# Moving a PSUM copy ahead of an absolute value on ScalarE, and VectorE's half of an outer product directly behind a difference

## The chip, the cores and the metric

The program runs on one core of a Trainium2 chip. The metric is the device time of one execution in microseconds; three executions of the kernel before were timed and one more was profiled.

## The reference

Three stages follow each other on 6016 tokens (two batches of 3008) of width 256:

```python
X = np.fft.fft(np.fft.fft(x, axis=1), axis=2).real      # x: (2, 3008, 256)
h = X.reshape(6016, 256) @ w_in1;  g = np.maximum(h, 0.0) ** 2;  z = g @ w_out1    # w_in1: (256, 2048)
h = z @ w_in2                                                                       # w_in2: (256, 2048)
P = a[0] + a[1] * h + a[2] * h**2 + a[3] * h**3
Q = 1.0 + np.abs(b[0]) * np.abs(h) + np.abs(b[1]) * h**2
out = (P / (Q + 1e-6)) @ w_out2                                                     # (6016, 256)
```

## The kernel before

**Stages.** The first 70 us or so transform the input: a DFT in two factors (`stage1`, `stage3`), with the DFT over the width folded into the first weight matrix. From there on the kernel is one pipeline of STEPS = 96 steps. The tokens are columns; a tile holds 256 column pairs (k and its mirror image), which are 512 columns of the output, and there are 12 tiles, the last one narrower (196 pairs, 392 columns). Each tile has 8 units of the hidden width, a unit being two blocks of 128 of the 2048 hidden features. A step handles one unit in each of four matrix products, skewed against each other: in step s, TensorE does `up1(s)` (first layer up), `down1(s - 2)`, `up2(s - 10)` (second layer up) and `down2(s - 12)`. Every product is done with values split in a high and a low part (`_hi`, `_lo`), three matmuls for one.

**The first layer and its mirror image.** For the column k and its mirror image the hidden value is a plus part plus or minus a minus part. `up1` computes the minus part into one PSUM bank (`h1_minus`, L901) and the plus part into another (`h1_plus`, L909). The plus part has one more term, an outer product of a row of the transform (`u_s`) with a weight column (`w_col`), which is not computed by TensorE: it is written into the plus bank first, and TensorE's plus matmuls add to it. The bank holds two blocks of 256 columns. In the first 12 steps (SHARED = SKEW + 2 = 12) VectorE writes both blocks (L707); afterwards ScalarE writes the second (L555) and VectorE the first. PSUM has one plus bank and one minus bank, so the outer product of unit s + 1 can be written only when VectorE has read the plus bank of unit s (`diff_done`).

**ScalarE's order in a step s** (from step 12 on; every operation is 128 partitions x 1024 columns unless another size is given): relu (L562) and square (L564) of unit s; its half of the outer product of s + 1 (L555, 256 columns); at the end of a tile, the high part of z (L619); |v| (L580) and the cubic term (L588) of the second layer's unit s - 10, both read from PSUM; the high part of g1 (`keep_hi1`, L571); at the end of a tile, the copy of the output out of PSUM (L626); |q'| (`abs_q`, L594), which needs VectorE's q'; the copy of the minus part of unit s + 1 (`keep_minus`, L547, 512 columns); the natural logarithm (L604) and the exponential (L607), which make the seed of the reciprocal of Q. The logarithm waits for |q'| by a semaphore, the exponential for the logarithm.

**VectorE's order in a step s**: sum (L735) and difference (L736) of unit s, from the plus bank and the copied minus part, 512 columns each; the division of unit s - 11 (`divide`: L753, L755, L759, the first one waits for the seed); its half of the outer product of s + 1 (L707); at the end of a tile, the low part of z (L764); then `read_h2` of unit s - 10 (L742 makes the signed q' and waits for ScalarE's two results; L743 and L745 make the polynomial and free the PSUM banks of `up2`).

**GpSimd's order**: high (L501) and low part (L503) of the divided g2, then the low part of g1 (`keep_lo1`, L494).

Every engine runs its program in the order written, and stands still at a wait. The waits that the change touches: VectorE's outer product waited for ScalarE's half of the same unit (`act_outer_ready`), ScalarE's for the difference of the unit before; TensorE's plus matmuls waited for VectorE's half (`outer_ready`), and so for both. The DMAs of these steps (the tile's inputs from DRAM, the output) are issued by SyncE's queue once per tile.

Of the kernel before, what the change touches and what calls it, by code (L numbers as in the profile page):

```python
# [64 lines left out]
SHARED = SKEW + 2  # L65
# [67 lines left out]
def fft_moe_kernel(nc, x, w_in1, w_out1, w_in2, w_out2, coef, f47, fold, twiddle, pair, out_t):  # L133
# [9 lines left out]
    with ctx:  # L143
# [105 lines left out]
        def unit(m):  # L249

            return m if 0 <= m < STEPS else None
# [265 lines left out]
        def _(act):  # L517
# [31 lines left out]
            def outer_product(m):  # L549
                t, n = m // UNITS, pairs(m // UNITS)  # L550
                f = 2 * (m % UNITS) + 1
                if m % UNITS == 0:
                    act.wait_ge(u_loaded[t % Y_BUFS], 16 * (t // Y_BUFS + 1))
                act.wait_ge(diff_done, m)
                nc.scalar.activation(h1_plus(m)[:, 1, :], u_s[:, t % Y_BUFS, 0:n], ACT.Copy, scale=w_col[:, f:f + 1]  # L555
                                     ).then_inc(act_outer_ready, 1)

# [82 lines left out]
            for s in range(STEPS):  # L640
                second, summed, multiplied = unit(s - SKEW), unit(s - LAG1), unit(s - SKEW - LAG2)
                square_relu(s)
                if SHARED <= s + 1 < STEPS:
                    outer_product(s + 1)
                if summed is not None and summed % UNITS == UNITS - 1:
                    keep_z_hi(summed // UNITS)
                if second is not None:
                    from_h2(second)
                if s >= HEAD:
                    keep_hi1(s)  # L650
                if multiplied is not None and multiplied % UNITS == UNITS - 1:
                    keep_out(multiplied // UNITS)
                if second is not None:
                    abs_q(second)
                if unit(s + 1) is not None:
                    keep_minus(s + 1)
                if s == 0:
                    keep_y_hi(EARLY)
                if second is not None:
                    seed_from_q(second)  # L660
                if s < HEAD:
                    keep_hi1(s)
                if s == 0:
                    keep_y_hi(EARLY + 1)
# [19 lines left out]
        def _(dve):  # L684
# [13 lines left out]
            def outer_product(m):  # L698
                t, n = m // UNITS, pairs(m // UNITS)
                if m % UNITS == 0:  # L700
                    dve.wait_ge(u_loaded[t % Y_BUFS], 16 * (t // Y_BUFS + 1))
                after(dve, diff_done, m)
                if m >= SHARED:
                    dve.wait_ge(act_outer_ready, m + 1 - SHARED)
                for i in range(2 if m < SHARED else 1):
                    f = 2 * (m % UNITS) + i
                    nc.vector.tensor_scalar(h1_plus(m)[:, i, :], u_s[:, t % Y_BUFS, 0:n], w_col[:, f:f + 1], None, ALU.mult  # L707
                                            ).then_inc(outer_ready, 1)
# [68 lines left out]
            for s in range(STEPS):  # L777
                second, before, summed = unit(s - SKEW), unit(s - SKEW - 1), unit(s - LAG1)
                add_and_subtract(s)
                if before is None:  # L780
                    outer_product(s + 1)
                if s == 1:
                    keep_y_lo(EARLY)
# [3 lines left out]
                    keep_y_lo(EARLY + 1)  # L787
                if before is not None:
                    divide(before)
                if before is not None and unit(s + 1) is not None:  # L790
                    outer_product(s + 1)
                if summed is not None and summed % UNITS == UNITS - 1:
                    keep_z_lo(summed // UNITS)
                if second is not None:
# [8 lines left out]
            m = STEPS - 1  # L803
# [10 lines left out]
        def _(pe):  # L814
# [74 lines left out]
            def up1(m):  # L889
# [12 lines left out]
                                                start=(i == 0 and (a, c) == (1, 0)), stop=(a, c) == (0, 0),  # L902
                                                skip_group_check=True)
                last.then_inc(minus_ready, 1)
                pe.wait_ge(outer_ready, 2 * m + 2 if m < SHARED else SHARED + m + 1)
                for i in range(2):
                    f = slice((2 * (m % UNITS) + i) * P, (2 * (m % UNITS) + i + 1) * P)
                    for a, c in ((1, 0), (0, 1), (0, 0)):
# [106 lines left out]
```

## Time and profile before

| | before |
|---|---|
| median of three runs | 1044.67 us (1043.86 to 1045.47) |
| the profiled execution's own time | 1044.86 us |
| its span in the trace | 1043.1 us |
| TensorE matmul / VectorE / ScalarE / GpSimd busy | 1005.7 / 919.0 / 913.4 / 573.0 us |
| granted TensorE clock, mean | 0.995 |

The span runs from the first to the last recorded instruction; the time of the execution is somewhat longer. Busy shares are means over the whole span, and a matmul's end is modelled, so TensorE's busy time does not say how far it is from its own limit. A row of the timeline gives the start of an instruction, its duration, and in brackets how long its engine stood idle before it and for whom. An instruction's recorded duration overlaps with the start of the next one on its engine, so the distance between two starts is what an instruction takes of its engine's time.

### The profile page before, as it was taken

Reading aid. Unit: us, or ns where it says so; the run is one execution under the profiler, and the core shown is the slowest. Engines: PE = TensorE matmul, PEld = TensorE weight load, DVE = VectorE, ACT = ScalarE, POOL = GpSimd, SP = SyncE. Lnnn points to the kernel's source line nnn. Section 1 sums busy time; section 2 is a strip of 40 time slices with the busy share of each in tenths; the row PEclk is TensorE's granted clock in tenths of the full one; section 3 lists DMA queues with packets and bytes.
Section 4 is the critical chain, followed back from the end, with each engine's and each line's share of the span. In section 5 each row is a group of like instructions: output and inputs, shape, how many; then the busy total and the mean of one; then the engine's idle time right before and its main releaser. Section 6 shows DMA issues by size and latency. Waiting matters only on the chain.

```text
span 1043.1 us, 13795 instructions
## 1 busy us (share of the span) xinstructions
PE 1005.7 (96%) x5098; PEld 840.4 (81%) x5098; DVE 919.0 (88%) x956; ACT 913.4 (88%) x1013; POOL 573.0 (55%) x305
## 2 busy tenths in 40 slices
PE   9999899999999999999999999999999999999975
PEld 8798778888888888888888888788788788888864
DVE  2369899999999999999999999989999999999997
ACT  2348899999999999999999999999999999999873
POOL 0246765655655656556556565565565655655352
PEclk9999999999999999999999999999999999999998
DMA  9767000001001001001001001001001000000000
GB/s 259 276 194 232 11 1 26 1 1 47 1 1 46 1 1 46 1 1 46 1 1 46 1 1 46 1 1 46 1 1 40 1 1 21 1 21 1 1 20 16
DMA packets 24992, 38.03 MB, mean 36 GB/s; under 512 B 1743, under 2 KB 19035, under 8 KB 24539
## 3 DMA queue, kind: packets, MB, share of 16 engines
q1 hardware_dynamic: 24876, 37.14, 11.3%
q8 instruction: 40, 0.66, 0.3%
q14 instruction: 28, 0.22, 0.1%
q10 hardware_dynamic: 48, 0.02, 0.0%
HBM read 25.31 MB, written 11.84 MB: 36 GB/s over the span
## 4 chain that ended last, share of the span: by engine, by line
ACT 55%; PE 16%; DVE 16%; issue 11%; ACTq 0%; DVEq 0%
DVE den_s L742 9%; ACT g_value L588 8%; ACT seed_s L604 8%; ACT g_value L562 8%; ACT seed_s L607 7%; ACT den_s L580 7%; ACT g_value L564 7%; PE ps L885 6%; ACT minus_s L547 4%; PE ps L876 3%; PE ps L822 3%; ACT ps L555 2%; PE ps L842 2%; PE ps L831 1%; ACT den_s L594 1%
## 5 line engine op out<-in xcount | busy, mean ns | idle before, releaser
L885 PE MATMUL ps<-g_hi,w_out_lo 128*128 128x512 f32 (+1 forms) x764 | 300.1, 393 | 18.9 <-POOL w_in_lo L503 8.3
L885 PE MATMUL ps<-g_hi,w_out_hi 128*128 128x512 f32 (+1 forms) x764 | 299.4, 392 | 0.0
L885 PE MATMUL ps<-g_lo,w_out_hi 128*128 128x512 f32 (+1 forms) x728 | 283.9, 390 | 0.0
L501 POOL CAST g_hi<-g_value 128x1024 fp32r<-128x1024 f32 x86 | 89.5, 1041 | 346.8 <-DVE g_value L759 346.8
L503 POOL TENSOR_TENSOR g_lo<-g_value,g_hi 128x1024 fp32r<-128x1024 f32 x86 | 208.1, 2419 | 6.9
L494 POOL TENSOR_TENSOR g_lo<-g_value,g_hi 128x1024 fp32r<-128x1024 f32 (+1 forms) x86 | 203.7, 2369 | 1.2 <-ACT g_hi L571 1.2
L885 PEld LDWEIGHTS ps<-g_hi,w_out_lo 128*128 128x128 f32 x764 | 145.3, 190 | 49.1 <-POOL w_in_lo L503 9.8
L885 PEld LDWEIGHTS ps<-g_hi,w_out_hi 128*128 128x128 f32 x764 | 144.6, 189 | 29.2
L885 PEld LDWEIGHTS ps<-g_lo,w_out_hi 128*128 128x128 f32 x728 | 137.8, 189 | 25.6
L742 DVE SCALAR_TENSOR_TENSOR den_s<-den_s,b_abs,ps 128x1024 f32<-128x1024 f32 x88 | 112.7, 1280 | 31.3 <-ACT g_value L588 31.3
L753 DVE SCALAR_TENSOR_TENSOR den_s<-den_s,seed_s 128x1024 f32<-128x1024 f32 x87 | 107.2, 1232 | 28.4 <-ACT seed_s L607 28.4
L594 ACT ACTIVATE den_s<-den_s 128x1024 f32<-128x1024 f32 x88 | 93.5, 1062 | 38.0 <-DVE den_s L742 38.0
L876 PE MATMUL ps<-z_hi,w_in_lo 128*128 128x512 f32 x352 | 115.1, 408 | 9.1 <-DVE g_value L745 8.2
L759 DVE SCALAR_TENSOR_TENSOR g_value<-g_value,coef_s,den_s 128x1024 f32<-128x1024 f32 x86 | 110.5, 1285 | 3.0
L745 DVE SCALAR_TENSOR_TENSOR g_value<-g_value,coef_s,ps 128x1024 f32<-128x1024 f32 x86 | 110.2, 1281 | 3.0
L876 PE MATMUL ps<-z_lo,w_in_hi 128*128 128x512 f32 x352 | 109.3, 392 | 0.0
L755 DVE SCALAR_TENSOR_TENSOR den_s<-den_s,seed_s 128x1024 f32<-128x1024 f32 x87 | 106.6, 1225 | 3.0
L876 PE MATMUL ps<-z_hi,w_in_hi 128*128 128x512 f32 x352 | 108.8, 390 | 0.0
L562 ACT ACTIVATE g_value<-g_value 128x1024 f32<-128x1024 f32 (+1 forms) x96 | 100.1, 1043 | 7.5 <-DVE g_value L736 7.5
L743 DVE TENSOR_TENSOR g_value<-g_value,ps 128x1024 f32<-128x1024 f32 x86 | 104.4, 1214 | 0.0
L564 ACT ACTIVATE g_value<-g_value 128x1024 f32<-128x1024 f32 (+1 forms) x96 | 100.4, 1046 | 3.0
L607 ACT ACTIVATE seed_s<-seed_s,exp_bias 128x1024 f32<-128x1024 f32 x87 | 100.4, 1154 | 2.8
(119 smaller groups left out, 1895.3 us busy)
## 6 DMA issues: line engine op xcount, KB each, us to landing
x_s<-x SPq DMA_DIRECT2D x16, 384.0 KB, 6.7
out_t<-out_s SPq DMA_DIRECT2D x11, 512.0 KB, 5.8
w_out_unsplit_lo<-w_out SPq DMA_DIRECT2D x2, 2048.0 KB, 17.3
tw_s<-twiddle SPq DMA_DIRECT2D x1, 3012.0 KB, 17.1
y_hi_dram<-y_stage_hi SPq DMA_DIRECT2D x10, 256.0 KB, 3.7
y_lo_dram<-y_stage_lo SPq DMA_DIRECT2D x10, 256.0 KB, 4.5
w_in_raw<-w_in SPq DMA_DIRECT2D x1, 2048.0 KB, 9.7
w_in_unsplit_lo<-w_in SPq DMA_DIRECT2D x4, 512.0 KB, 5.9
```

Of the source, the lines that this page charges most:

```text
L494: nc.gpsimd.tensor_tensor(g1_lo_s[:, p, :, 0:n], r_s[:, p, :, 0:n], g1_hi_s[:, m % 2, :, 0:n].bitcast(F32), ALU.subtract).then_inc(pool_lo ...
L503: nc.gpsimd.tensor_tensor(lo, g, hi.bitcast(F32), ALU.subtract).then_inc(g2_lo, 1)
L562: nc.scalar.activation(r, r, ACT.Relu).then_inc(relu_done, 1)
L564: nc.scalar.activation(r, r, ACT.Square).then_inc(g1_done, 1)
L607: nc.scalar.activation(seed, seed, ACT.Exp, bias=exp_bias[:, 0:1], scale=-1.0).then_inc(seed_done, 1)
L742: nc.vector.scalar_tensor_tensor(den, den, b_abs[:, 0:1], h2, ALU.add, ALU.mult).then_inc(q_signed, 1)
L745: nc.vector.scalar_tensor_tensor(num, num, a1, h2, ALU.add, ALU.mult).then_inc(h2_read, 1)
L753: nc.vector.scalar_tensor_tensor(den, den, Q_CONST, seed, ALU.add, ALU.mult).then_inc(t_done, 1)
L755: nc.vector.scalar_tensor_tensor(den, den, 2.0, seed, ALU.subtract, ALU.mult, reverse0=True).then_inc(rec_done, 1)
L759: nc.vector.scalar_tensor_tensor(num, num, a0, den, ALU.add, ALU.mult).then_inc(g2_done, 1)
L876: last = nc.tensor.matmul(h[:, i, 0:n], lhs, rhs, start=(j == 0), stop=(j == len(products) - 1))
L885: last = nc.tensor.matmul(acc[:, mb, 0:n], w[a][:, f, mb * P:(mb + 1) * P], g[c][:, i, 0:n], start=(f == 0 and j == 0), stop=(f == FB - 1 ...
```

## The change

ScalarE copies the minus part of the next unit ahead of |q'|, and no longer between |q'| and the logarithm. VectorE writes its half of the next unit's outer product directly behind the difference in every step, as it did in the first steps only, and no longer behind the division; it doesn't wait for ScalarE's half any more. ScalarE's half waits for VectorE's half, and TensorE's plus matmuls wait for ScalarE's half once there is one. No operation is added, removed or resized.

```diff
--- before.py
+++ after.py
@@ -551,7 +551,7 @@
                 f = 2 * (m % UNITS) + 1
                 if m % UNITS == 0:
                     act.wait_ge(u_loaded[t % Y_BUFS], 16 * (t // Y_BUFS + 1))
-                act.wait_ge(diff_done, m)
+                act.wait_ge(outer_ready, SHARED + m + 1)
                 nc.scalar.activation(h1_plus(m)[:, 1, :], u_s[:, t % Y_BUFS, 0:n], ACT.Copy, scale=w_col[:, f:f + 1]
                                      ).then_inc(act_outer_ready, 1)
 
@@ -650,10 +650,10 @@
                     keep_hi1(s)
                 if multiplied is not None and multiplied % UNITS == UNITS - 1:
                     keep_out(multiplied // UNITS)
+                if unit(s + 1) is not None:
+                    keep_minus(s + 1)
                 if second is not None:
                     abs_q(second)
-                if unit(s + 1) is not None:
-                    keep_minus(s + 1)
                 if s == 0:
                     keep_y_hi(EARLY)
                 if second is not None:
@@ -700,8 +700,6 @@
                 if m % UNITS == 0:
                     dve.wait_ge(u_loaded[t % Y_BUFS], 16 * (t // Y_BUFS + 1))
                 after(dve, diff_done, m)
-                if m >= SHARED:
-                    dve.wait_ge(act_outer_ready, m + 1 - SHARED)
                 for i in range(2 if m < SHARED else 1):
                     f = 2 * (m % UNITS) + i
                     nc.vector.tensor_scalar(h1_plus(m)[:, i, :], u_s[:, t % Y_BUFS, 0:n], w_col[:, f:f + 1], None, ALU.mult
@@ -777,7 +775,7 @@
             for s in range(STEPS):
                 second, before, summed = unit(s - SKEW), unit(s - SKEW - 1), unit(s - LAG1)
                 add_and_subtract(s)
-                if before is None:
+                if unit(s + 1) is not None:
                     outer_product(s + 1)
                 if s == 1:
                     keep_y_lo(EARLY)
@@ -787,8 +785,6 @@
                     keep_y_lo(EARLY + 1)
                 if before is not None:
                     divide(before)
-                if before is not None and unit(s + 1) is not None:
-                    outer_product(s + 1)
                 if summed is not None and summed % UNITS == UNITS - 1:
                     keep_z_lo(summed // UNITS)
                 if second is not None:
@@ -902,7 +898,10 @@
                                                 start=(i == 0 and (a, c) == (1, 0)), stop=(a, c) == (0, 0),
                                                 skip_group_check=True)
                 last.then_inc(minus_ready, 1)
-                pe.wait_ge(outer_ready, 2 * m + 2 if m < SHARED else SHARED + m + 1)
+                if m < SHARED:
+                    pe.wait_ge(outer_ready, 2 * m + 2)
+                else:
+                    pe.wait_ge(act_outer_ready, m + 1 - SHARED)
                 for i in range(2):
                     f = slice((2 * (m % UNITS) + i) * P, (2 * (m % UNITS) + i + 1) * P)
                     for a, c in ((1, 0), (0, 1), (0, 0)):
```

## Rows read from the trace of the kernel before

**Rows 1.** The page's chain that ended last, by engine, shares of the span.
```profile
ACT 55%; PE 16%; DVE 16%; issue 11%; ACTq 0%; DVEq 0%
```

**Rows 2.** The list of waits: total us, times, longest us.
```profile
ACT den_s L594 <- DVE den_s L742: 38.0, 76, 0.7
```

**Rows 3.** Timeline of one ordinary step: start, duration, engine, line, operation, idle before.
```profile
522.67 2.42 POOL L494 TENSOR_TENSOR g_lo<-g_value,g_hi 128x1024 fp32r<-128x1024 f32 x1
...
521.21 1.06 ACT L594 ACTIVATE den_s<-den_s 128x1024 f32<-128x1024 f32 x1 [0.48 <-DVE den_s L742]
522.18 0.58 ACT L547 ACTIVATE minus_s<-ps 128x512 f32<-128x512 f32 x1
522.65 1.14 ACT L604 ACTIVATE seed_s<-den_s,ln_bias 128x1024 f32<-128x1024 f32 x1
...
524.92 1.06 ACT L562 ACTIVATE g_value<-g_value 128x1024 f32<-128x1024 f32 x1
...
528.38 1.19 ACT L588 ACTIVATE g_value<-ps,coef_s 128x1024 f32<-128x1024 f32 x1
...
519.90 1.28 DVE L742 SCALAR_TENSOR_TENSOR den_s<-den_s,b_abs,ps 128x1024 f32<-128x1024 f32 x1 [0.40 <-ACT g_value L588]
...
524.15 0.68 DVE L736 TENSOR_TENSOR g_value<-ps,minus_s 128x512 f32<-128x512 f32 x1
525.09 1.23 DVE L753 SCALAR_TENSOR_TENSOR den_s<-den_s,seed_s 128x1024 f32<-128x1024 f32 x1 [0.27 <-ACT seed_s L607]
...
529.69 1.28 DVE L742 SCALAR_TENSOR_TENSOR den_s<-den_s,b_abs,ps 128x1024 f32<-128x1024 f32 x1 [0.39 <-ACT g_value L588]
```

**Rows 4.** Timeline of an early step, before the second layer has begun.
```profile
84.23 0.68 DVE L736 TENSOR_TENSOR g_value<-ps,minus_s 128x512 f32<-128x512 f32 x1
84.94 0.87 DVE L707 TENSOR_SCALAR ps<-u_s,w_col 128x256 f32<-128x256 f32 x2
...
85.00 1.06 ACT L562 ACTIVATE g_value<-g_value 128x1024 f32<-128x1024 f32 x1 [0.52 <-DVE g_value L736]
```

**Rows 5.** Timeline of ScalarE in a step with the copy of out_s.
```profile
529.47 1.05 ACT L571 ACTIVATE g_hi<-g_value 128x1024 fp32r<-128x1024 f32 x1
530.42 1.03 ACT L626 ACTIVATE out_s<-ps 128x1024 f32<-128x1024 f32 x1
531.32 1.06 ACT L594 ACTIVATE den_s<-den_s 128x1024 f32<-128x1024 f32 x1
...
532.75 1.16 ACT L604 ACTIVATE seed_s<-den_s,ln_bias 128x1024 f32<-128x1024 f32 x1
...
535.00 1.05 ACT L562 ACTIVATE g_value<-g_value 128x1024 f32<-128x1024 f32 x1
```

**Rows 6.** Timeline of TensorE soon after down2 has begun, and that step's L742.
```profile
142.30 1.28 DVE L742 SCALAR_TENSOR_TENSOR den_s<-den_s,b_abs,ps 128x1024 f32<-128x1024 f32 x1 [0.76 <-ACT g_value L588]
...
143.09 0.28 PE L901 MATMUL ps<-y_odd_hi,w_in_hi 128*128 128x256 f32 x1
...
156.42 0.62 PE L876 MATMUL ps<-z_hi,w_in_lo 128*128 128x512 f32 x2
...
166.12 0.62 PE L876 MATMUL ps<-z_hi,w_in_lo 128*128 128x512 f32 x2
```

**Rows 7.** Timeline of ScalarE in the last step, where nothing stands between |q'| and ln.
```profile
963.29 1.06 ACT L594 ACTIVATE den_s<-den_s 128x1024 f32<-128x1024 f32 x1 [0.69 <-DVE den_s L742]
964.38 1.16 ACT L604 ACTIVATE seed_s<-den_s,ln_bias 128x1024 f32<-128x1024 f32 x1
```

**Rows 8.** Timeline of a step of the narrow last tile, TensorE and ScalarE.
```profile
922.12 0.62 PE L876 MATMUL ps<-z_hi,w_in_hi 128*128 128x512 f32 x2
...
922.83 1.10 ACT L580 ACTIVATE den_s<-ps,coef_s 128x1024 f32<-128x1024 f32 x1
```

**Rows 9.** Timeline of GpSimd and VectorE in a step where the two overlap.
```profile
711.66 2.42 POOL L494 TENSOR_TENSOR g_lo<-g_value,g_hi 128x1024 fp32r<-128x1024 f32 x1
...
713.72 1.45 DVE L753 SCALAR_TENSOR_TENSOR den_s<-den_s,seed_s 128x1024 f32<-128x1024 f32 x1 [0.27 <-ACT seed_s L607]
```

## The prediction

> **What bounds the kernel now.** I read first the page's chain of work that ended last [rows 1]: 55% of the span is ScalarE, 16% each VectorE and TensorE. The list of waits [rows 2] names ScalarE's largest idle time: 38.0 us in front of |q'| (L594), 76 times, until VectorE's signed q' (L742) is there. Read that way, work slid into this idle time is time gained. The timeline of one ordinary step [rows 3] says otherwise, and it is the view to trust, because it gives distances.
>
> Let T be the start of L742. In the step at T = 519.90 the next L742 starts at 529.69: the step takes 9.79 us. ScalarE: |q'| at T+1.31 (L742 lasts 1.28, then 0.03), the minus copy (L547) at T+2.28, ln T+2.75, relu T+5.02, the cubic term T+8.48; the next L742 starts 1.31 after the cubic. VectorE: the difference starts at T+4.25. So relu starts 0.77 after the difference starts, and 2.27 after ln.
>
> Which of the two holds relu? In the first steps, where ScalarE stands idle 0.52 us for the difference, relu starts 0.77 after the difference's start as well [rows 4]. That is the distance when VectorE holds it. In the step that also copies out_s, ln to relu is 2.25 [rows 5], less than the 2.27 of the ordinary step; that is the distance when ScalarE's own order holds it. So in the ordinary step both ways end at relu within 0.02 us, and VectorE's is the later one. Relu's row shows no idle time, since the exp before it still runs when relu can start; the distances alone tell it. The loop that sets the step is then L742, the rest of read_h2, the sum and the difference on VectorE (4.25), the hand-over (0.77), and relu, square, the outer half, |v| and the cubic on ScalarE up to the next L742 (529.69 - 524.92 = 4.77): 4.25 + 0.77 + 4.77 = 9.79. Neither |q'|, the minus copy, ln nor exp is in it.
>
> TensorE stands close behind: where it is late and waits for nothing, its second layer's groups (L876) follow each other in 166.12 - 156.42 = 9.70 us [rows 6].
>
> **The change, part by part.**
>
> *Minus copy ahead of |q'|.* It keeps its length. The copy of g_hi (L571) starts at T-0.22 (529.47 against 529.69), and the next Activate behind it comes 0.95 later [rows 5], so the copy can start at T+0.73. It needs TensorE's minus group: the latest in the wide steps is that of the step at T = 142.30, whose last matmul starts at 143.09 and lasts 0.28 [rows 6], T+1.07. There the copy would start near T+1.1. TensorE's 9.70 gains 0.09 a step on the 9.79, so the following groups end earlier each time. It holds its engine 0.47 (522.65 - 522.18), so |q'| starts at T+1.31 as now in an ordinary step, and at about T+1.6 in that late one. Behind |q'| stands ln, which waits for it: where these two are neighbours already, they start 1.09 apart [rows 7], against 0.97 from |q'| to the minus copy [rows 3]. ln then starts at T+2.40 instead of T+2.75, and ScalarE reaches relu at T+2.40+2.25 = T+4.65, 0.37 earlier than relu starts now. In the late step it reaches it at T+4.95, still ahead of T+5.02. Relu stays at T+5.02, held by the difference. Worth in the 57 ordinary steps of the wide tiles (s = 12 to 86 are 75, less nine with the z copy and nine with the out_s copy): 0. The z copy lies between the outer half and |v|, in the loop and behind relu, so those nine steps keep their length too. The cover that hides the reorder is 0.37 us in each step; without it the 0.12 lost on ln would be paid 75 times, 9 us.
>
> *The ten steps with the out_s copy.* Here ScalarE is the bound: |q'| starts at 531.32, T+1.63, with no idle in front, and relu at T+5.31, where the difference would allow T+5.02 [rows 5]. The order becomes out_s, minus, |q'|, ln: the minus copy still takes its 0.47, but |q'| to ln costs 1.09 instead of the 0.95 or 0.97 to the minus copy. From |q'| to ln these rows show 532.75 - 531.32 = 1.43; after the change minus and |q'| take 0.47 + 1.09 = 1.56. Each such step becomes 0.13 us longer: 10 x 0.13 = **+1.3 us**. Bounds: 0, if an Activate that waits for its predecessor starts no later than one that doesn't; 0.2 if the copy of PSUM in front of |q'| overlaps less than it does in front of ln.
>
> The Trainium skill speaks to this term: "ScalarE: Activation LUTs", section "What ACT_TABLE_LOAD costs", has Activates back to back overlap by about 93 ns and makes no exception for one that reads the other's result. By that rule the ten steps would cost nothing. Rows 7 disagree with it: |q'| lasts 1.06 and ln starts 1.09 after it.
>
> *VectorE's half directly behind the difference.* In the first steps it already stands there: L707 starts 0.71 after the difference, and relu keeps its 0.77 [rows 4]. So it doesn't delay the hand-over. One half is about 0.44 (0.87 for two), so L753 can start at T+4.25+0.71+0.44 = T+5.40; it now starts at T+5.19, 2.44 after ln, and the seed will be there at T+2.40+2.44 = T+4.84. The division slides 0.2 us later, but at its end 0.44 us of the outer half are gone, so VectorE comes free for the next L742 0.2 us earlier than now. L742 waits for the cubic, not for VectorE: worth 0. GpSimd's split of g2 starts 0.2 later; it is used by down2 in a later step. The wait on TensorE for both halves is met at the latest when ScalarE's half ends, about T+7.6, and its first-layer plus group starts only after the next T. ScalarE's half, which now waits for VectorE's, runs at about T+7.1, and VectorE's is done by T+5.4. Nothing queues behind these waits. No DMA is moved.
>
> *The narrow last tile* (from s = 87). The difference works on 392 instead of 512 columns there, so it holds relu less, and the shorter way to relu may count. But |v| starts at 922.83, and TensorE's last pair of matmuls for it is recorded from 922.12 to 922.74 [rows 8]; with 0.03 for the hand-over, as in front of |q'|, it can gain 0.06 in a step at most. I take three steps of this kind, since the others have the z or the out_s copy, or |v| waits for TensorE already: -0.15 us, between -0.5 (0.06 in all eight) and 0.
>
> Sum: 0 + 1.3 - 0.15 = +1.15 us. The profiled execution took 1044.86 for a span of 1043.1; that makes it 1046.0, and on the median of 1044.67, 0.19 below it, **1045.8 us**.
>
> **Rivals.**
>
> *A, ScalarE holds the step, as the page's chain says.* Then relu would come at T+4.65, the loop would be 9.42, and TensorE's 9.70 would hold: 57 x 0.09 = 5.1 us, the nine z steps 0.37 each, 3.3 us, less the 1.3: 7.1 us, 1037.6 us. For it: 0.02 us is little to decide on. Against: the 0.77 that ordinary and first steps share. Chance 0.08.
>
> *B, the minus copy takes the wait of |q'| over (slower).* The copy stands in front of |q'| and waits for TensorE. With 0.37 us of cover behind T+1.31 it costs nothing while the minus group ends before about T+1.14 (T+1.14 + 0.04 + 0.47 = T+1.65 for |q'|). Against: the latest in the wide steps is T+1.07, and the others come earlier. For: a matmul's end is modelled, and its semaphore may come later than it. From T+1.14 on each 0.1 counts in full: with groups at T+1.24 in all 57 steps it is 5.7 us on top of the 1.15, 1051.5 us. Chance 0.05.
>
> *C, VectorE's division runs into GpSimd.* GpSimd's g_lo (L494) starts at 522.67 and lasts 2.42: it ends at T+5.19, as L753 starts [rows 3]. Where L753 began 0.36 before that end it took 1.45 instead of 1.23 [rows 9]. L753 and L494 now slide together by the same 0.2, so I expect no overlap; if it comes, it decides only when VectorE is over 0.7 late for L742 (from T+5.40, L753 to L759 and its slot are 3.7, so T+9.1 against 9.79). Price with 0.9 late in 57 steps: 0.2 x 57 = 11 us, 1057 us. Chance 0.03. This is the rule of the Trainium skill's "SBUF — State Buffer", section "Who interferes with whom": a VectorE instruction with two SBUF inputs contends with a GpSimd one that reads SBUF. By that rule, the trace agrees with the 1.45.
>
> *D, dependent Activates cost nothing extra*, the lower bound above: 1044.67 - 0.15 = 1044.5 us. Chance 0.08.
>
> **How the numbers follow.** My forecast has the remaining 0.76. No change can be told from one within 0.2% of 1044.67, 2.1 us either way. Forecast and D lie within it; for the copy's upper bound (0.2 x 10) and the spread of the runs shown, 0.8 either way, I take 0.05 of the forecast as slower and 0.01 as faster. Faster: 0.08 + 0.01 = 0.09. Slower: 0.05 + 0.03 + 0.05 = 0.13. Same: 0.78. The range takes in D with its spread and the low end of the last tile, 1044.67 - 0.5 - 0.8 = 1043.4, and the upper bound, 1044.67 + 2.0 + 0.8 = 1047.5; A, B and C, 0.16, stay outside.
>
> **What would show it.** In the changed profile the idle time in front of |q'| shrinks to about 0.1 us a step, and idle time in front of relu until L736 appears, 0.3 to 0.4 us in some 66 steps: the stall has moved. L742 to L742 stays 9.79 in ordinary steps, and goes up by 0.13 to about 10.2 (5.44 + 4.77) with the out_s copy. ln starts 1.09 after |q'|. The idle time in front of L753 goes. Wrong is this if ordinary steps are shorter than 9.77 (A) or longer than 9.81 (B, with idle time in front of L547; C, with L742 starting right behind L759).

## The result, and the profile after

| | before | after |
|---|---|---|
| median | 1044.67 us (13 runs, 1043.73 to 1045.81) | 1046.76 us (13 runs, 1045.16 to 1048.04) |
| the profiled execution's own time | 1044.86 us | 1047.46 us |
| its span | 1043.1 us | 1045.7 us |
| TensorE matmul / VectorE / ScalarE / GpSimd busy | 1005.7 / 919.0 / 913.4 / 573.0 us | 1009.1 / 919.1 / 928.0 / 572.7 us |
| granted TensorE clock, mean | 0.995 | 0.991 |

The ratio is 1.0019, with a 95% interval of 1.0010 to 1.0028. By the bound of 0.2% that counts as no change, but only just: the whole interval lies above 1, and its upper end above the bound. The kernel has become about 2 us slower, where 1.1 us was forecast. A second measurement of the same two kernels gave 1.0016 (1.0007 to 1.0025), so the small loss is real. Below, T is again the start of the instruction that makes the signed q' (L742 before, L740 after; the line numbers of VectorE's and TensorE's code move up by two to four).

The page's chain that ended last and two rows of the list of waits, of the kernel after:

```profile
ACT 37%; DVE 30%; PE 19%; issue 13%; ACTq 0%; DVEq 0%
```

```profile
DVE den_s L740 <- ACT g_value L588: 53.3, 85, 3.6
ACT g_value L562 <- DVE g_value L734: 25.9, 78, 2.1
```

ScalarE's 38.0 us of idle time in front of |q'| [rows 2] is gone from the list. In its place relu (L562) waits for the difference (L734), 25.9 us in 78 steps, and the chain has moved from 55% ScalarE [rows 1] to 37% ScalarE and 30% VectorE. Not much of the time has gone with it. The timeline of an ordinary step of the kernel after, ScalarE and then VectorE (start, duration, engine, line, operation, idle before):

```profile
519.01 1.20 ACT L588 ACTIVATE g_value<-ps,coef_s 128x1024 f32<-128x1024 f32 x1
520.10 1.05 ACT L571 ACTIVATE g_hi<-g_value 128x1024 fp32r<-128x1024 f32 x1
521.05 0.59 ACT L547 ACTIVATE minus_s<-ps 128x512 f32<-128x512 f32 x1
521.63 1.06 ACT L594 ACTIVATE den_s<-den_s 128x1024 f32<-128x1024 f32 x1
522.73 1.15 ACT L604 ACTIVATE seed_s<-den_s,ln_bias 128x1024 f32<-128x1024 f32 x1
523.91 1.15 ACT L607 ACTIVATE seed_s<-seed_s,exp_bias 128x1024 f32<-128x1024 f32 x1
525.34 1.06 ACT L562 ACTIVATE g_value<-g_value 128x1024 f32<-128x1024 f32 x1 [0.27 <-DVE g_value L734]
...
520.32 1.28 DVE L740 SCALAR_TENSOR_TENSOR den_s<-den_s,b_abs,ps 128x1024 f32<-128x1024 f32 x1 [0.63 <-ACT g_value L588]
...
524.56 0.68 DVE L734 TENSOR_TENSOR g_value<-ps,minus_s 128x512 f32<-128x512 f32 x1
525.28 0.49 DVE L705 TENSOR_SCALAR ps<-u_s,w_col 128x256 f32<-128x256 f32 x1
525.67 1.22 DVE L751 SCALAR_TENSOR_TENSOR den_s<-den_s,seed_s 128x1024 f32<-128x1024 f32 x1
...
530.10 1.28 DVE L740 SCALAR_TENSOR_TENSOR den_s<-den_s,b_abs,ps 128x1024 f32<-128x1024 f32 x1 [0.63 <-ACT g_value L588]
```

The step takes 530.10 - 520.32 = 9.78 us, as before [rows 3]. Its loop has the same three parts: the difference starts at T+4.24, relu 0.78 after it, and the next T comes 4.76 after relu. ScalarE's side has changed as meant: the minus copy fills the wait, |q'| starts at T+1.31 as ever, ln at T+2.41 instead of T+2.75, 1.10 after |q'|. All that it buys is that relu, which ScalarE's own order would now reach at about T+4.66, stands idle until T+5.02. The row shows 0.27 of that idle and not 0.36, because the recorded duration of the exp (1.15) runs on beyond the point at which the next Activate could start: in the out_s step, where relu waits for nothing, it starts 1.06 after the exp (the rows in experiment 3).

**The lengths of the steps**, start of one q' to start of the next, taken from the timelines of the two profiles:

| steps | before | after | difference |
|---|---|---|---|
| step 10, from the first q' to the second | 9.77 | 9.78 | +0.01 |
| step 11 | 10.16 | 9.78 | -0.38 |
| 57 ordinary steps of the wide tiles | 557.87 (median 9.79) | 558.02 (median 9.78) | +0.15 |
| of these, step 81 | 9.79 | 10.13 | +0.34 |
| nine steps with the z copy | 96.29 (10.70) | 96.32 (10.70) | +0.03 |
| nine steps with the out_s copy, wide tiles | 90.54 (10.06) | 91.83 (10.20) | +1.29 |
| eight steps of the last tile (87 to 94), the tenth out_s copy among them | 74.97 | 75.04 | +0.07 |
| sum | 839.60 | 840.77 | +1.17 |

The other 1.4 us of the 2.6 between the two spans lie outside: 0.33 in front of the first q' (a time that goes from 121.4 to 123.1 over the profiles of this study, whatever the kernel) and 1.10 behind the last one.

### The profile page after: what moved, and what is told of

Read it like the earlier page. It is cut to its first block, busy times and chain, and to the rows that moved or that the text cites. A ratio compares the mean times of both kernels' runs of the same rounds, so it can differ in the third digit from the quotient of the medians.

```text
span 1045.7 us, 13721 instructions
## 1 busy us (share of the span) xinstructions
PE 1009.1 (97%) x5098; PEld 843.4 (81%) x5098; DVE 919.1 (88%) x956; ACT 928.0 (89%) x1013; POOL 572.7 (55%) x305
## 4 chain that ended last, share of the span: by engine, by line
ACT 37%; DVE 30%; PE 19%; issue 13%; ACTq 0%; DVEq 0%
DVE den_s L740 8%; ACT g_value L588 8%; ACT g_value L562 8%; ACT g_value L564 7%; ACT den_s L580 7%; DVE g_value L741 7%; PE ps L881 7%; DVE g_value L733 4%; DVE g_value L734 4%; PE ps L872 4%; PE ps L818 3%; PE ps L838 2%; PE ps L827 1%; ACT seed_s L604 1%; PE ps L908 1%
## 5 line engine op out<-in xcount | busy, mean ns | idle before, releaser
L740 DVE SCALAR_TENSOR_TENSOR den_s<-den_s,b_abs,ps 128x1024 f32<-128x1024 f32 x88 | 112.7, 1280 | 53.4 <-ACT g_value L588 53.3
L562 ACT ACTIVATE g_value<-g_value 128x1024 f32<-128x1024 f32 (+1 forms) x96 | 100.2, 1044 | 25.9 <-DVE g_value L734 25.9
L743 DVE SCALAR_TENSOR_TENSOR g_value<-g_value,coef_s,ps 128x1024 f32<-128x1024 f32 x86 | 110.2, 1281 | 3.0
L753 DVE SCALAR_TENSOR_TENSOR den_s<-den_s,seed_s 128x1024 f32<-128x1024 f32 x87 | 106.6, 1225 | 3.0
L604 ACT ACTIVATE seed_s<-den_s,ln_bias 128x1024 f32<-128x1024 f32 x87 | 100.4, 1154 | 2.8
```

The source lines that it names most:

```text
L562: nc.scalar.activation(r, r, ACT.Relu).then_inc(relu_done, 1)
L604: nc.scalar.activation(seed, den, ACT.Ln, bias=ln_bias[:, 0:1], scale=2.0 ** -LN_SHIFT).then_inc(ln_done, 1)
L740: nc.vector.scalar_tensor_tensor(den, den, b_abs[:, 0:1], h2, ALU.add, ALU.mult).then_inc(q_signed, 1)
L743: nc.vector.scalar_tensor_tensor(num, num, a1, h2, ALU.add, ALU.mult).then_inc(h2_read, 1)
L753: nc.vector.scalar_tensor_tensor(den, den, 2.0, seed, ALU.subtract, ALU.mult, reverse0=True).then_inc(rec_done, 1)
```

## The experiments

The tests that were timed in repeated runs stand in one table, each with the kernel before beside it on the same chip; the others were run once. The last column gives the median ordinary step and the usual out_s step of the one profile of each.

| kernel | median us | before us | ratio (95%) | ordinary / out_s step |
|---|---|---|---|---|
| VectorE's half alone | 1044.63 | 1045.38 | 0.9995 (0.9987 to 1.0004) | 9.79 / 10.06 |
| minus copy alone | 1045.47 | 1045.38 | 1.0003 (0.9994 to 1.0012) | 9.79 / 10.20 |
| the change, out_s steps in the old order | 1045.48 | 1045.38 | 1.0000 (0.9991 to 1.0009) | 9.79 / 10.05 |
| that, and ScalarE's half behind the cubic | 1032.56 | 1045.38 | 0.9881 (0.9866 to 0.9896) | 9.69 / 9.66 |
| the kernel before once more | 1045.29 | 1045.09 | 1.0001 (0.9992 to 1.0010) | 9.79 / 10.06 |
| the change once more | 1046.62 | 1045.09 | 1.0016 (1.0007 to 1.0025) | 9.79 / 10.20 |
| the change and four small memsets | 1046.13 | 1044.72 | 1.0014 (1.0005 to 1.0023) | 9.79 / 10.21 |

**1. VectorE's half alone.** The change with ScalarE's old order:

```diff
-                if unit(s + 1) is not None:
-                    keep_minus(s + 1)
                 if second is not None:
                     abs_q(second)
+                if unit(s + 1) is not None:
+                    keep_minus(s + 1)
```

> The changed kernel with ScalarE's minus copy back between |q'| and ln: only VectorE's half of the outer product is moved. My theory: relu is held by VectorE's difference, so ordinary steps stay at 9.79 us and steps with the out_s copy stay at 10.06; the only change is step 11, where the trace of the changed kernel shows 9.78 in place of 10.16, since TensorE no longer waits 4.1 us for VectorE's half. Time -0.4 us against before, ratio 0.9996. Rival (the move of VectorE's half is what costs): steps with the out_s copy at 10.20 here too, time about +1.2.

Its out_s steps are back at 10.06 and its ordinary steps are 9.79: moving the half costs these steps nothing, and the loss in the out_s steps is not from it. Step 11 took 9.78, as expected. Two single steps of its profile are longer, 12 (10.75) and 81 (10.16); experiment 7 takes them up.

**2. The minus copy alone.** The kernel before with ScalarE's new order:

```diff
-                if second is not None:
-                    abs_q(second)
                 if unit(s + 1) is not None:
                     keep_minus(s + 1)
+                if second is not None:
+                    abs_q(second)
```

> The kernel before with the minus copy ahead of |q'| and nothing else moved. My theory: ordinary steps 9.79, the ten steps with the out_s copy 10.20 (9.45 in the last tile) instead of 10.06 (9.30), step 11 at 10.16 as before; time +1.4 us from the steps, and up to +1 more if TensorE's clock at the very end falls as in the changed kernel. Rival (ScalarE holds the step, so that the filled idle time counts): ordinary steps below 9.77 and a time of -5 or less.

Two rows of its list of waits:

```profile
DVE den_s L742 <- ACT g_value L588: 51.1, 82, 2.7
ACT g_value L562 <- DVE g_value L736: 25.2, 76, 2.1
```

The wait has moved to relu with this half of the change alone, and the nine out_s steps take 91.79 us together, 1.25 more than before, the step with the tenth one 9.46 instead of 9.31. So both what the change shows in the waits and what it costs in the out_s steps come from the order on ScalarE. Step 11 missed its expectation: 10.59 us and not 10.16, with |v| waiting 0.71 us for TensorE. In the other profiles with both halves in their old places this step took 10.16, 10.08 and, with the pad of experiment 4, 9.97, so it varies, and no run shows that the copy did this. The time of whole executions does not resolve this sum of 1.4 us (1.0003, with 0.9 us either way); the step lengths, which repeat to 0.01 us, do.

**3. The change, but the old order in the out_s steps.**

```diff
+                out_step = multiplied is not None and multiplied % UNITS == UNITS - 1
+                if out_step:
+                    abs_q(second)
                 if unit(s + 1) is not None:
                     keep_minus(s + 1)
-                if second is not None:
+                if second is not None and not out_step:
                     abs_q(second)
```

> The changed kernel, but in the ten steps with the out_s copy the order is |q'|, minus, ln as before. My theory: those steps return to 10.06, everything else as in the changed kernel: 1.4 us less than the changed kernel from the steps, so -0.4 against before plus whatever TensorE's clock at the end does. Rival (the loss of the changed kernel lies elsewhere, in the drain): steps at 10.06 but the time stays 1 us or more above before.

The out_s steps are 10.05, the ratio is 1.0000. In these steps relu comes directly behind the exp in either order (of the kernel after):

```profile
530.10 1.28 DVE L740 SCALAR_TENSOR_TENSOR den_s<-den_s,b_abs,ps 128x1024 f32<-128x1024 f32 x1 [0.63 <-ACT g_value L588]
...
531.74 0.60 ACT L547 ACTIVATE minus_s<-ps 128x512 f32<-128x512 f32 x1
532.21 1.07 ACT L594 ACTIVATE den_s<-den_s 128x1024 f32<-128x1024 f32 x1
533.31 1.16 ACT L604 ACTIVATE seed_s<-den_s,ln_bias 128x1024 f32<-128x1024 f32 x1
534.50 1.16 ACT L607 ACTIVATE seed_s<-seed_s,exp_bias 128x1024 f32<-128x1024 f32 x1
535.56 1.05 ACT L562 ACTIVATE g_value<-g_value 128x1024 f32<-128x1024 f32 x1
```

Relu starts at T+5.46, with no idle in front, against T+5.31 [rows 5]. From the copy behind out_s to ln it is 533.31 - 531.74 = 1.57 where it was 1.43: |q'| and the ln that waits by a semaphore for its result and reads it start 1.10 apart; with the copy between them, which depends on neither, it was 0.97 from |q'| to the copy and 0.47 from the copy to ln [rows 3]. The Trainium skill's "ScalarE: Activation LUTs", section "What ACT_TABLE_LOAD costs", says that Activates back to back overlap by about 93 ns; the independent pairs here do (1.06 long, 0.97 apart), the pair of which one reads the other's result does not, and the ten steps measured it.

**4. One, or four, more Activates in front of relu.** If VectorE's difference holds relu by 0.37 us in the changed kernel, work of less than that in front of relu is free there and dear in the kernel before. In both kernels one copy of 160 columns into a scratch tile was added behind the exp of every step that has a |q'| and no out_s copy (the same edit in both):

```diff
+        pad_s = sb("pad_s", [P, 160])
...
                     seed_from_q(second)
+                out_step = multiplied is not None and multiplied % UNITS == UNITS - 1
+                if second is not None and unit(s + 1) is not None and not out_step:
+                    act.wait_ge(minus_kept, s + 2)
+                    for _ in range(1):
+                        nc.scalar.activation(pad_s[:, :], minus_s[:, 0, 0:160], ACT.Copy)
```

> The changed kernel with one more Activate of 160 columns behind exp, in every step that has |q'| and no out_s copy (a copy into a tile that nobody reads). It takes about 0.15 to 0.2 us of ScalarE, by the spacing of the 512- and 1024-column ones. My theory: ScalarE reaches relu 0.37 before the difference allows it, so ordinary steps stay at 9.79. Rival (ScalarE's own order holds the step): 0.15 to 0.2 more in every ordinary step, 10 us in all.

> The same additional Activate in the kernel before, where ScalarE reaches relu only 0.02 before the difference allows it: ordinary steps grow by nearly all of it, 0.13 to 0.18 us each, to 9.92 to 9.97; 9 to 12 us in all. If the minus copy's move had made no cover, both kernels would grow alike.

Two consecutive q' of the changed kernel with the pad, and the same of the kernel before with it:

```profile
520.73 1.28 DVE L746 SCALAR_TENSOR_TENSOR den_s<-den_s,b_abs,ps 128x1024 f32<-128x1024 f32 x1 [0.64 <-ACT g_value L589]
...
530.51 1.28 DVE L746 SCALAR_TENSOR_TENSOR den_s<-den_s,b_abs,ps 128x1024 f32<-128x1024 f32 x1 [0.63 <-ACT g_value L589]
```

```profile
516.29 1.28 DVE L748 SCALAR_TENSOR_TENSOR den_s<-den_s,b_abs,ps 128x1024 f32<-128x1024 f32 x1 [0.36 <-ACT g_value L589]
...
526.25 1.28 DVE L748 SCALAR_TENSOR_TENSOR den_s<-den_s,b_abs,ps 128x1024 f32<-128x1024 f32 x1 [0.56 <-ACT g_value L589]
```

9.78 against 9.96. The changed kernel with the pad took 1047.93 us, the one before with it 1057.95, which is 12.9 above the median before where 9 to 12 had been expected. In the kernel before the 57 ordinary steps add up to 567.94, 10.07 more than without; the rest lies mostly in the z steps (10.88) and in the last tile. Relu there had next to no room: the pad puts it 0.20 later in ScalarE's order, and the step grows by 0.18. A larger pad finds the end of the room in the changed kernel: four copies of 40 columns each in place of the one.

```diff
-                    for _ in range(1):
-                        nc.scalar.activation(pad_s[:, :], minus_s[:, 0, 0:160], ACT.Copy)
+                    for n in range(4):
+                        nc.scalar.activation(pad_s[:, n * 40:n * 40 + 40], minus_s[:, 0, n * 40:n * 40 + 40], ACT.Copy)
```

> The changed kernel with four Activates of 40 columns each behind exp instead of one of 160. One took 0.175 in the kernel before; four short ones take about 0.5, more than the 0.37 of cover. My theory: ordinary steps grow by the excess, 0.10 to 0.20, to 9.89 to 9.99. Rival (the cover is larger, or the steps are bound elsewhere): 9.79.

The four copies of this kernel, and the q' behind them with the one of the next step:

```profile
508.78 0.60 ACT L666 ACTIVATE pad_s<-minus_s 128x40 f32<-128x40 f32 x4
...
514.94 1.28 DVE L746 SCALAR_TENSOR_TENSOR den_s<-den_s,b_abs,ps 128x1024 f32<-128x1024 f32 x1 [0.53 <-ACT g_value L589]
...
524.85 1.28 DVE L746 SCALAR_TENSOR_TENSOR den_s<-den_s,b_abs,ps 128x1024 f32<-128x1024 f32 x1 [0.75 <-ACT g_value L589]
```

They hold ScalarE for 0.50 us up to relu at 509.28, and the step is 9.91: 0.13 longer than the 9.78 of the changed kernel. 0.50 - 0.13 = 0.37 is the room, the number that the prediction worked out as T+5.02 less T+4.65.

**5. ScalarE's half of the outer product behind the cubic term.** If the loop is difference, relu, square, outer half, |v|, cubic, q', then the way to gain is to take the outer half out of it. Experiment 3 with one more edit (the out_s steps, where ScalarE holds relu, keep the old place):

```diff
                 square_relu(s)
-                if SHARED <= s + 1 < STEPS:
+                out_step = multiplied is not None and multiplied % UNITS == UNITS - 1
+                if SHARED <= s + 1 < STEPS and out_step:
                     outer_product(s + 1)
...
                     from_h2(second)
+                if SHARED <= s + 1 < STEPS and not out_step:
+                    outer_product(s + 1)
                 if s >= HEAD:
```

> As minus_not_in_out_steps, and ScalarE's half of the outer product stands behind the cubic term instead of ahead of |v|, except in steps with the out_s copy. It takes 0.40 us out of the loop that I hold for the bound (difference, relu, square, outer half, |v|, cubic, L740). My theory: that loop falls to 9.39, so TensorE's 9.70 takes over: ordinary steps 9.70 (57 x 0.09 = 5.1 us), steps with the z copy 10.30 (9 x 0.40 = 3.6 us), steps behind the out_s copy up to 0.35 shorter (9 times, 3.2 us): 1033 us, -11 us. If relu were not in the loop (ScalarE's whole order is the bound) the move would not change the sum of ScalarE's order and the time stays within 1 us of before.

It took 1032.56 us (4 runs, 1030.73 to 1034.1) beside 1045.38 before, 12.8 less, and beats both kernels. By the steps: the ordinary ones 548.87 instead of 557.87, the out_s ones 86.94 instead of 90.54. First the page's chain of this kernel, then its timeline around one q' and the next, VectorE and then ScalarE:

```profile
PE 86%; DVE 7%; ACT 4%; issue 3%; ACTq 0%; DVEq 0%
```

```profile
541.84 1.28 DVE L745 SCALAR_TENSOR_TENSOR den_s<-den_s,b_abs,ps 128x1024 f32<-128x1024 f32 x1 [0.18 <-ACT g_value L588]
...
551.53 1.28 DVE L745 SCALAR_TENSOR_TENSOR den_s<-den_s,b_abs,ps 128x1024 f32<-128x1024 f32 x1 [0.24 <-ACT g_value L588]
...
547.95 1.06 ACT L564 ACTIVATE g_value<-g_value 128x1024 f32<-128x1024 f32 x1
549.20 1.12 ACT L580 ACTIVATE den_s<-ps,coef_s 128x1024 f32<-128x1024 f32 x1 [0.19 <-PE ps L877]
550.22 1.20 ACT L588 ACTIVATE g_value<-ps,coef_s 128x1024 f32<-128x1024 f32 x1
551.30 0.48 ACT L555 ACTIVATE ps<-u_s,w_col 128x256 f32<-128x256 f32 x1
```

The step is 9.69, the 9.70 at which TensorE's groups followed each other where it was late [rows 6], and |v| (L580) waits for TensorE. The bound has passed to TensorE: of the 0.39 that the outer half took from ScalarE, 0.10 is gained in an ordinary step. Only in the step behind a z copy, which gives TensorE time to get ahead (10.66), is the whole of it gained, 9.39; behind an out_s step it is 9.48, and the nine steps in front of an out_s step, where the half keeps its old place, stay at 9.79. The sum came out near the expected 11, but not where it was expected: the z steps were given 10.30 and took 10.66, since the z copy itself now waits for TensorE (0.24 us at 500.27), and the gain came in the step behind them.

**6. The same move without the change.** ScalarE's half behind the cubic, the same edit made in the kernel before, where VectorE's half still stands behind the division and waits for ScalarE's.

> The kernel before with only ScalarE's half moved behind the cubic term, as in outer_behind_cubic, but VectorE's half still behind the division and waiting for it. The loop loses 0.40 on ScalarE, but VectorE's half must now wait for ScalarE's at about T+9.6 and L742 stands behind it: ordinary steps about 10.1, steps with the z copy about 12.1, 25 to 30 us slower. So the move of VectorE's half, worth nothing by itself, would be what makes the 11 us of outer_behind_cubic possible. Rival (it isn't needed): 1033 us here too.

1083.42 us in one run, 38.7 more than the median before, against the 25 to 30 that were expected. The ordinary step (10.13) and the z step (12.18) came as expected; the out_s steps (10.41) and the last tile (79.32 instead of 74.97) had not been counted. Its timeline over one step, VectorE, then ScalarE:

```profile
496.80 1.27 DVE L745 SCALAR_TENSOR_TENSOR den_s<-den_s,b_abs,ps 128x1024 f32<-128x1024 f32 x1
...
506.56 0.49 DVE L710 TENSOR_SCALAR ps<-u_s,w_col 128x256 f32<-128x256 f32 x1 [0.78 <-ACT ps L555]
506.96 1.27 DVE L745 SCALAR_TENSOR_TENSOR den_s<-den_s,b_abs,ps 128x1024 f32<-128x1024 f32 x1
...
504.86 1.20 ACT L588 ACTIVATE g_value<-ps,coef_s 128x1024 f32<-128x1024 f32 x1
505.95 0.47 ACT L555 ACTIVATE ps<-u_s,w_col 128x256 f32<-128x256 f32 x1
```

VectorE's half waits for ScalarE's, and q' stands behind it on VectorE: the half is in the loop again, with a hand-over of 0.61 on top, and q' starts 2.10 after the cubic instead of 1.31. The ordinary step is 10.13 (10.16 here). In experiment 5, where VectorE's half has been written long before, this wait is gone. So VectorE's half directly behind the difference, worth nothing by itself, is what takes this wait out of the way of experiment 5. The two kernels differ in the order of the minus copy as well, and the two halves moved without it were not run together; the rows name VectorE's half and not the copy.

**7. Where the rest of the 2 us comes from: the kernels once more, and four memsets.** The kernel before and the changed one were timed a second time, without an edit:

> The kernel before, unchanged, so that its clock records can be set against those of the changed kernel, beside which it runs. The profiled runs differ by 1.1 us behind the last L742 of the pipeline (end minus that start: 81.1 before, 82.2 changed), where TensorE's last 24 matmuls ran at the lower clock for 4.1 us more. If that were an effect of the change, all runs of before would show a mean granted clock near 0.995 and all of the changed one 0.990 to 0.992. If it falls by chance with the run, both kernels show the same spread of clocks and their medians lie 1.1 us apart from the steps alone (1.4 for the out_s copy, +0.3 for one stall of VectorE, -0.4 in step 11, -0.2 rest).

> The changed kernel, unchanged, beside the kernel before on the same chip: steps as in its first profile (9.79, 10.70, 10.20, step 81 with 0.34 more), time +1.1 us by the steps; +2.1 if the clock at the end belongs to the change.

The kernel before gave 1.0001 against itself, the changed one 1.0016. In the profile of the first measurement step 81 had cost 0.34. VectorE stalls there in front of the q' that ends the step, although the cubic that it waits for had started in time. The q' that begins this step and the late one:

```profile
829.01 1.28 DVE L740 SCALAR_TENSOR_TENSOR den_s<-den_s,b_abs,ps 128x1024 f32<-128x1024 f32 x1 [0.42 <-ACT g_value L588]
...
839.14 1.28 DVE L740 SCALAR_TENSOR_TENSOR den_s<-den_s,b_abs,ps 128x1024 f32<-128x1024 f32 x1 [0.98 <-ACT g_value L588]
```

The cubic of that step starts at 837.49, so q' comes 1.65 after it instead of 1.31. The same q' is late, by 0.34 to 0.37, in all seven profiles of kernels in which VectorE has the program of the change, also in the one with four pads, where it comes at 847.07 instead of 839.14: the stall keeps to the instruction and not to the time. In the same stretch, 836 to 841 us, the DMA view has this row (packets, MB, share of the 16 engines) for the queue that carries instructions:

```profile
q14 instruction: 2, 0.02, 0.9%
```

The same view has no packet from 836 to 839.2 us: both come only after the late q' has started (839.14), so they stand beside the stall and are not shown to cause it.

Four memsets of one column each, ahead of VectorE's first work, shift its program by four instructions and nothing else:

```diff
+        pad_s = sb("pad_s", [P, 8])
...
+            for n in range(4):
+                dve.memset(pad_s[:, n:n + 1], 0.0)
             for g in range(1, S1_GROUPS, 2):
```

> The changed kernel with four more VectorE memsets of one column at the very start, into a tile that nobody reads; they shift every later VectorE instruction by four places in the program. In three profiles of kernels with VectorE's half moved, step 81 takes 0.34 to 0.37 more, with L740 late though the cubic was there, and packets of the queue that loads instructions near it; before, a stall of the same size stands in front of L753 in step 69, where VectorE has room. If the stall belongs to a place in the program, it now strikes four instructions earlier, in the division, where VectorE has 0.7 us of room: step 81 takes 9.79 and the time falls by 0.3. If it belongs to a moment of the run or to chance, step 81 stays long or another is.

The same two q' of this kernel (L743 here):

```profile
830.02 1.28 DVE L743 SCALAR_TENSOR_TENSOR den_s<-den_s,b_abs,ps 128x1024 f32<-128x1024 f32 x1 [0.42 <-ACT g_value L589]
...
839.81 1.28 DVE L743 SCALAR_TENSOR_TENSOR den_s<-den_s,b_abs,ps 128x1024 f32<-128x1024 f32 x1 [0.64 <-ACT g_value L589]
```

9.79: q' is no longer late. The stall is tied to a place in VectorE's program, not to the work of the step. Where it went is open: the expectation put it into the division, whose rows in this step start 1.25 and 1.26 us apart as in the others. In the profile before, an idle time longer than usual by the same amount (0.62 instead of 0.27) stood in front of L753 at 704.27, where VectorE has room. The time of the kernel (1.0014) does not tell 0.3 us apart.

The repeated profile of the change shows what is larger. In step 12 it took 10.71 instead of 9.79. TensorE waits there, once, and then runs at its lower clock. The windows view of the repeated kernel and of the first profile of the change over the same 6 us (length, busy times with counts, granted clock, DMA share, GB/s), and then a matmul row of the repeated kernel:

```profile
144.00:150.00 6.00, 4.91 (x15) 3.96 (x16) 5.89 (x7) 4.80 (x6) 2.57 (x2) 0.72 0.00 0
```

```profile
144.00:150.00 6.00, 5.11 (x22) 3.88 (x22) 5.89 (x7) 5.62 (x7) 3.59 (x2) 1.00 0.00 0
```

```profile
145.09 1.22 PE L872 MATMUL ps<-z_hi,w_in_lo 128*128 128x512 f32 x2 [2.20 <-DVE g_value L743]
...
149.68 1.12 ACT L580 ACTIVATE den_s<-ps,coef_s 128x1024 f32<-128x1024 f32 x1 [0.85 <-PE ps L872]
```

TensorE had been idle for 2.20 us, the clock went from 2.4 to 1.2 GHz, two matmuls of 512 columns took 1.22 instead of 0.62 [rows 6], and |v| waited 0.85 for them. In every profile of this study that has VectorE's half moved and ScalarE's half in its old place (seven of them), TensorE first waits 2.26 us in step 11 (2.38 in the one with four pads); in four the clock falls right behind that wait and steps 11 and 12 take the length of an ordinary step, in the other three it stays at 2.4 GHz, falls in step 12 instead, and that step costs 0.9 more. The wait of 2.20 us belongs to the other three alone: where the clock had fallen in step 11, TensorE comes later to this place and waits 0.78 to 0.97 us there.

## Why the prediction came out as it did

**What bounds the kernel: right, and shown.** The loop of 4.25 + 0.77 + 4.77 held relu in the kernel before, although no row showed a wait there. The change took 38.0 us of recorded idle time out of ScalarE and no ordinary step became shorter; the pads found 0 and 0.37 us of room in front of relu, before and after; and the only edit that shortened the step was the one that took an operation out of the loop. That is the end of rival A (1037.6 us).

**The out_s steps: right in place and size.** +0.13 each was forecast, +0.14 measured: nine steps 1.29, and the tenth 0.15 (9.31 and 9.46 in the repeated profiles). Rival D (dependent Activates cost nothing extra) falls with it, by experiments 1 to 3.

**The minus copy's wait for TensorE (rival B)** came in eight steps, three before the second layer begins and five in the last tile, 2.6 us in all, and held nothing up. (By the prediction's own numbers the copy is free up to T+5.02-2.25-1.09-0.47-0.04 = T+1.17, and not T+1.14; nothing hung on it.) **VectorE's division against GpSimd (rival C)** came only in two steps of the last tile (1.44 and 1.40 us), at no cost. In the kernel of experiment 2, where the division was not moved 0.2 us back, it came in the wide steps behind out_s as well (1.45 at 227.41), and cost nothing there either. **The z steps** stayed at 10.70. **The last tile** was given -0.15 and gained 0.08 beside the 0.15 of its out_s step.

**VectorE's half: the term 0 was mis-sized, at the start.** The prediction put the wait of TensorE on both halves at nothing for the steady steps, where it is nothing. At the start of the second layer, in front of step 11, TensorE had run out of other work and its plus matmuls did wait for the halves. The kernel before, then the kernel after:

```profile
131.82 0.39 PE L909 MATMUL ps<-y_odd_hi,w_in_lo 128*128 128x256 f32 x1 [4.14 <-DVE ps L707]
```

```profile
130.29 0.58 PE L908 MATMUL ps<-y_odd_hi,w_in_lo 128*128 128x256 f32 x1 [2.26 <-ACT ps L555]
```

1.88 us less idle, of which 0.38 reached the step (10.16 to 9.78; 10.08 to 9.78 in the repeated profiles). In the three profiles where the clock falls a step later it is taken back with 0.5 more: 0.9 - 0.38.

**What was not in the sum.** That the steps add up to +1.17, as good as the forecast's +1.15, is luck in part: step 11 (-0.38) and the stall of step 81 (+0.34) were in no term of it, and cancel. Of the 1.0 us between the forecast (1045.8) and the median (1046.76), the stall of step 81 is 0.34 in the profile. The clock of step 12, 0.9 in three of seven profiles, would be 0.4 on the mean if timed runs split in the same way; that is an estimate, since timed runs have no steps to look at. 1.17 + 0.4 = 1.6 us, against measured differences of 2.1 and 1.5 with 0.9 either way. The end of the kernel adds a third one to the first profile. Its last stretch, before and after:

```profile
1020.00:1043.00 23.00, 11.90 (x48) 10.73 (x48) 17.49 (x21) 7.94 (x10) 6.37 (x5) 0.85 0.05 17
```

```profile
1021.00:1045.70 24.70, 14.45 (x48) 13.28 (x48) 17.85 (x22) 7.94 (x10) 6.50 (x5) 0.70 0.04 17
```

The same 48 matmuls with a granted clock of 0.85 and 0.70: TensorE waits there three times for GpSimd and VectorE, 1.9 to 3.4 us each, and runs part of this stretch at 1.2 GHz, for longer in the one profile than in the other. From the last q' to the end it took 81.13 and 82.23 in the two profiles, 80.94 and 81.30 in the repeated ones, and 80.17 to 82.17 in the others: it spreads by 2.0 us in kernels with VectorE's half in its old place and in kernels with it moved, so the 1.10 between the first two profiles is not shown to be an effect of the change.

**Open** is whether it varies in quite the same way for both kernels. The mean granted clock was 0.990 to 0.992 in all 24 runs of the change, while of the 32 runs of the kernel before in the session of the repeats six had 0.995; they took 1044.5 us on the mean, the other 26 1045.2. In the other two sessions seven more of 42 runs of the kernel before had it. Whether the change makes such runs rarer was not settled.

## What to carry to other kernels

An instruction that shows no wait can still be held by another engine: compare its distance to the presumed releaser with the same distance in a step where it plainly waits, and the distance to its predecessor with a step where it plainly doesn't, before pricing idle time as gain. Work slid into idle time that lies off the loop only makes room further on; the gain comes with the next edit, which must take an operation out of the loop itself, and then the next bound (here TensorE, 9.70) says how much of it is paid out. Two changes can each be worth nothing or a loss (0.9995 and +38.7 us here) and together, with the new order of the minus copy beside them, be worth 12.8 us, so a neutral change is worth keeping if it takes a wait out of the way of another.

## What had not been expected of the hardware

- Behind an Activate of 1024 columns that lasts 1.06 an independent one starts 0.97 later, one that waits for its result and reads it 1.10 later, and the difference is not recorded as idle time.
- VectorE stood still for 0.34 to 0.37 us in front of the same q' of its program in seven profiles, and no longer there with four more instructions at the start. The cause is not shown; the packets on the queue that carries instructions come after it.
- TensorE's clock after an idle time of 2.26 us was 1.2 GHz in four profiles and 2.4 GHz in three, at the same place of practically the same program; where it fell there it cost nothing, and a step later it cost 0.9 us. Effects of this size are as large as the whole change.
- A copy of 40 columns took 0.12 to 0.13 us of ScalarE's time (0.50 for four), a copy of 160 columns some 0.2 (0.37 where relu was recorded behind it at its own wait).
